# A fused clustered-attention kernel: cluster ties through a triangular matmul, and the first lots and the first head in another order

## The chip, the cores and the metric

The program runs on one core of a Trainium2 chip. TensorE (PE), VectorE (DVE), ScalarE (ACT), GpSimd (POOL) and the sync engine (SP, which here only issues DMAs) each work through a queue of their own, in order, and wait for one another through semaphores. The metric is the device time of one execution in microseconds (us). The kernel before took 671.68 us, the median of three runs (670.71 to 671.84).

## The reference

Three stages in a row: attention of 2 batches x 8 heads x 768 tokens x 64, in which a query sees only the keys of its own cluster, and two MLPs over all 1536 tokens. Only the first stage is touched:

```python
q_assign = np.argmax(np.einsum('bhsd,hcd->bhsc', q_n, c_n), axis=-1)
k_assign = np.argmax(np.einsum('bhsd,hcd->bhsc', k_n, c_n), axis=-1)
mask = q_assign[:, :, :, None] == k_assign[:, :, None, :]
scores = scale * np.matmul(q, k.transpose(0, 1, 3, 2))
scores = np.where(mask, scores, -1000000000.0)
...   # softmax over the keys, then attn @ v, then the two MLPs
```

There are 16 clusters (C) for each head. `argmax` takes the first of equal values, so ties must be resolved the same way.

## The kernel before

Setup. The similarities of all tokens to the 16 centroids of their head are worked out in eight lots. Lot e belongs to batch e // 4, to q (x = 0) or k (x = 1), and to one half of the 768 tokens (c), for all 8 heads at once: 8 heads x 16 clusters fill the 128 partitions. A lot goes round the engines: SP loads it (`load_pairs`, 768 KB), PE multiplies it with the centroids (`sims_of`), ACT copies the result to SBUF (`copy_sims`), PE transposes it so that tokens lie on partitions (`tokens_of`), DVE takes each head's maximum over the 16 and marks who reaches it (`compare`), POOL multiplies the marks with a falling rank (`rank_lot`), DVE takes the maximum rank and marks the winner (`choose`). PE then turns two lots back at a time, clusters on partitions (`hots_of`), and ACT copies them into `hot_t` and scales them (`store_clusters`): 0 or 1 for q, 0 or -2^100 for k. These 16 rows per head are appended to q and k as extra contraction rows, so that the scores of pairs in different clusters become hugely negative.

A head. Each head's k and q (384 KB) are loaded (`load_kq`), scaled on POOL (`scale_q`), rounded to fp32r on ACT (`kq_high`), the remainder is taken on POOL (`kq_low`), and SP moves the parts to their partitions with small SBUF-to-SBUF DMAs (`place_head`): two out of `k_high`, one out of `k_low`, one within `k_high`, and last two with the cluster rows. When the last three have landed (`qk_ready`), PE may start on that head. For head 0 the cluster rows come straight from `hot_t`; for every other head they go through `mask_rows` in DRAM.

Attention. Two heads make a pair of 12 steps, one for each 128 query tokens; eight pairs follow one another, the first written out, the others in a loop. In step n PE makes the scores (`scores_of`, two banks in turn), DVE the row maximum (`row_max`), ACT the exponential (`exps`), POOL the normalisation, and five or six steps later PE transposes the result (`turn`), ACT and DVE split it (`turned_high`, `turned_low`), and PE multiplies it with v. In pair 0 the steps 0 to 5 have no such later work yet. The last two lots' `choose`, the last two `hots_of` and their `store_clusters` stand in steps 0 to 5 of pair 0, at the steps that `CHOOSE_STEPS`, `HOT_STEPS` and `STORE_STEPS` name. Before the first `turn` in step 6, PE waits until `hot_t` is complete, because the transposed probabilities use the same PSUM banks.

The order on each engine is the order in which the code is written; no scheduler moves anything.

Of the kernel before, what the change touches and what calls it, by code (L numbers as in the profile page):

```python
# [16 lines left out]
def clustered_attention_two_mlps(nc, q_t, k_t, v_r, cent, w_gelu, w_ln, gains, out):  # L17
# [32 lines left out]
    with ExitStack() as ctx:  # L50
# [32 lines left out]
        first_rank_i = sb("first_rank_i", [P, C], I32, cluster)  # L83
        first_rank = sb("first_rank", [P, C], F32, cluster)
# [6 lines left out]
        CHOICE_LAG = 1  # L91
        RANKS = CHOICE_LAG + 2
        sims_max = [sb(f"sims_max{r}", [P, CH * H], F32, cluster) for r in range(RANKS)]
        rank_max = [sb(f"rank_max{r}", [P, CH * H], F32, cluster) for r in range(RANKS)]
        rank = [sb(f"rank{r}", [P, HALF], F32, cluster) for r in range(RANKS)]
        hot = [sb(f"hot{x}", [P, S], F32, cluster) for x in range(2)]
        hot_t = [sb(f"hot_t{x}", [P, S], F32, cluster) for x in range(2)]
# [51 lines left out]
        sims_t_ps = [banks[:, 2 * x:2 * x + 2, 0:HALF] for x in range(2)]  # L149
        sims = [banks[:, 4 + c, 0:HALF] for c in range(2)]  # L150
        hot_ps = banks[:, 6:8, 0:HALF]
# [30 lines left out]
        ranked = sem("ranked")  # L182
        rank_max_done = sem("rank_max_done")
        hot_done = sem("hot_done")
        hot_ps_done = sem("hot_ps_done")
# [107 lines left out]
        KQ_STEP, STORE_STEPS, HOT_STEPS, CHOOSE_STEPS = 0, (2, 4), (3, 5), (0, 1)  # L293
# [42 lines left out]
        def _(sp):  # L336
            sp.dma_start(c_raw[:], cent).then_inc(cent_loaded, 16)
            sp.dma_start(gains_sb[:], gains).then_inc(gains_loaded, 16)

# [30 lines left out]
            def place_head(it, j):  # L370
# [16 lines left out]
                move(q_high[j][low, :], k_high[j][high, :], high_moved[j])  # L387
                if isinstance(it, int) and it == 0 and j == 0:

                    load_pairs(LOTS - 1)  # L390
                sp.wait_ge(kq_low_done, (h + 1) * 2)
                move(q_parts[j][high, :], k_low[j][high, :], low_moved[j])
# [23 lines left out]
            for j in range(2):  # L416
                load_v(0, j)
# [46 lines left out]
        def _(pe):  # L464
# [31 lines left out]
            def hots_of(g):  # L496
                pe.wait_ge(hot_done, (g + 1) * 2)
                if g >= 1:

                    pe.wait_ge(hot_t_done, g)  # L500
# [1046 lines left out]
```

## Time and profile before

| what | value |
|---|---|
| median of three runs | 671.68 us |
| profiled execution | 670.98 us, of it 669.1 us span |
| PE busy | 631.0 us (94%) |
| DVE / ACT / POOL busy | 485.1 / 325.1 / 494.1 us |
| first scores of pair 0 | 30.63 us after the start |
| first `turn` (step 6) of pair 0 | 42.57 us |
| first scores of pair 1 | 56.97 us |
| a pair in the middle of the loop | 27.3 us |

The profile gives, for one execution, when each instruction began, how long it took and what ended the idle time of its engine before it. All times are counted from the start of the span. The profiled execution's own time is 1.9 us above its span, for start and end. Everything from pair 1 on is untouched by the change, so the first 57 us decide.

### The profile page before, as it was taken

How to read it: one execution, taken by the hardware profiler on the slowest of the kernel's cores; microseconds unless marked ns; L12 is line 12 of the kernel's file. 1: busy time of each engine (PE TensorE's matmuls, PEld its weight loads, DVE VectorE, ACT ScalarE, POOL GpSimd, SP SyncE). 2: the span in 40 equal slices, each digit the busy share in tenths (PEclk: the TensorE clock that was granted, in tenths of full speed). 3: DMA queues.
4: the chain of work that ended last, by engine and by line, in shares of the span. 5: the costliest groups of instructions: out<-in, count | busy, mean ns of one | idle time of the engine just before them, and what ended most of it. 6: DMA issues, size and time to landing. Idle time of an engine off the chain costs nothing.

```text
span 669.1 us, 11407 instructions
## 1 busy us (share of the span) xinstructions
PE 631.0 (94%) x3245; PEld 528.5 (79%) x3245; DVE 485.1 (72%) x819; ACT 325.1 (49%) x647; POOL 494.1 (74%) x680
## 2 busy tenths in 40 slices
PE   4579999999999999999999999999999999999998
PEld 1369989898989888788877777788888877888876
DVE  3779999999999985666647667755555587778650
ACT  1279999999999984222222222132222243443341
POOL 2677788798888886888879888988887777567000
PEclk9889999999999999999999999999999999999999
DMA  8866544544545421232222222222220000000001
GB/s 283 266 176 145 158 120 112 143 123 126 143 112 137 134 88 64 72 110 88 106 96 82 84 88 91 94 95 96 94 94 31 1 0 17 32 17 17 31 33 47
DMA packets 26936, 64.31 MB, mean 96 GB/s; under 512 B 3872, under 2 KB 10016, under 8 KB 26912
## 3 DMA queue, kind: packets, MB, share of 16 engines
q1 hardware_dynamic: 24896, 60.09, 30.2%
q10 hardware_dynamic: 2016, 3.93, 1.6%
q8 instruction: 11, 0.18, 0.1%
q14 instruction: 13, 0.11, 0.1%
HBM read 46.60 MB, written 4.72 MB: 77 GB/s over the span
## 4 chain that ended last, share of the span: by engine, by line
PE 66%; ACT 11%; DVE 8%; issue 7%; DMA 4%; POOL 2%; DVEq 1%; SPq 1%; ACTq 0%; POOLq 0%
PE banks L560 6%; PE banks L575 6%; PE banks L577 6%; PE banks L590 6%; PE banks L576 6%; PE banks L592 6%; PE banks L591 6%; ACT probs L799 4%; PE banks L545 4%; PE banks L715 3%; PE banks L714 3%; PE banks L713 3%; ACT probs_th L810 2%; PE banks L682 2%; PE banks L684 2%
## 5 line engine op out<-in xcount | busy, mean ns | idle before, releaser
L1028 DVE TENSOR_TENSOR probs_tl<-banks,probs_th 128x384 fp32r<-128x384 f32 x192 | 100.4, 546 | 11.7 <-ACT probs_th L810 9.2
L1008 DVE TENSOR_REDUCE neg_max<-banks 128x1 f32<-128x768 f32 x96 | 91.0, 948 | 10.2 <-PE banks L532 8.4
L810 ACT CAST probs_th<-banks 128x384 fp32r<-128x384 f32 x192 | 83.0, 485 | 21.4 <-PE banks L545 20.0
L1337 POOL TENSOR_TENSOR wait_scrap<-half_power 128x1 f32<-128x1 f32 x176 | 47.2, 268 | 61.4 <-DVE row_inv L1022 29.6
L799 ACT ACTIVATE probs<-banks,neg_max 128x768 f32<-128x768 f32 x96 | 88.1, 918 | 7.6 <-DVE neg_max L1008 7.5
L1002 DVE TENSOR_TENSOR gl<-gate,gh 128x512 fp32r<-128x512 f32 x48 | 43.8, 912 | 65.1 <-ACT gh L784 65.1
L1413 POOL TENSOR_SCALAR probs<-probs,row_inv 128x768 f32<-128x768 f32 x96 | 87.7, 914 | 0.0
L545 PE MATMUL banks<-ident,probs 128*128 128x128 f32 x576 | 79.0, 272 | 0.9 <-ACT hot_t L753 0.9
L560 PE MATMUL banks<-probs_th,v_parts 128*128 128x384 f32 x192 | 70.3, 366 | 9.9 <-DVE x_sums L1035 9.9
L784 ACT CAST gh<-gate 128x512 fp32r<-128x512 f32 x48 | 29.8, 621 | 99.8 <-PE banks L592 58.7
L575 PE MATMUL banks<-xh,uph 128*128 (+1 forms) x192 | 76.7, 400 | 1.0 <-POOL upl L1386 0.8
L1396 POOL TENSOR_TENSOR downl<-gelu_raw,downh 128x512 fp32r<-128x512 f32 x48 | 73.8, 1537 | 4.0
L590 PE MATMUL banks<-gh,downh 128*128 128x512 f32 x192 | 75.9, 395 | 0.2
L577 PE MATMUL banks<-xh,upl 128*128 (+1 forms) x192 | 75.4, 392 | 0.0
L592 PE MATMUL banks<-gh,downl 128*128 128x512 f32 x192 | 75.3, 392 | 0.0
L576 PE MATMUL banks<-xl,uph 128*128 (+1 forms) x192 | 75.1, 391 | 0.0
L591 PE MATMUL banks<-gl,downh 128*128 128x512 f32 x192 | 74.8, 390 | 0.0
L545 PEld LDWEIGHTS banks<-ident,probs 128*128 128x128 f32 x576 | 68.5, 140 | 5.2 <-ACT hot_t L753 1.2
L1386 POOL TENSOR_TENSOR upl<-gelu_raw,uph 128x512 fp32r<-128x512 f32 x48 | 67.7, 1410 | 4.0
L780 ACT ACTIVATE gate<-banks 128x512 f32<-128x512 f32 x48 | 28.8, 599 | 84.8 <-PE banks L577 65.4
L560 PE MATMUL banks<-probs_tl,v_parts 128*128 128x384 f32 x192 | 65.1, 339 | 0.0
L528 PE MATMUL banks<-k_high,q_parts 128*128 128x384 f32 x192 | 56.4, 376 | 5.4 <-DMA k_low<-mask_rows 2.1
(147 smaller groups left out, 1410.7 us busy)
## 6 DMA issues: line engine op xcount, KB each, us to landing
gelu_raw<-w_gelu SPq DMA_DIRECT2D x48, 512.0 KB, 3.3
ln_raw<-w_ln SPq DMA_DIRECT2D x8, 512.0 KB, 4.7
pair_t<-q_t SPq DMA_DIRECT2D x4, 768.0 KB, 7.4
pair_t<-k_t SPq DMA_DIRECT2D x4, 768.0 KB, 8.3
kq_raw<-k_t SPq DMA_DIRECT2D x16, 192.0 KB, 3.7
kq_raw<-q_t SPq DMA_DIRECT2D x16, 192.0 KB, 3.9
q_parts<-k_high SPq DMA_DIRECT2D x16, 192.0 KB, 2.6
q_high<-k_high SPq DMA_DIRECT2D x16, 192.0 KB, 3.0
```

What stands on the lines that cost most here:

```text
L545: last = nc.tensor.transpose(pt_bank(n, c)[:, t * P:(t + 1) * P], probs[:, n % NP, k * P:(k + 1) * P], ident[:])
L560: last = nc.tensor.matmul(head_out, v_parts[j][:, i // 2].rearrange("p two d -> p (two d)"), part[half % 2][:, i // 2, :], start=i == 0, s ...
L575: nc.tensor.matmul(hidden[u], uph[u][:, cols], xh[:, k, tok], start=k == 0, stop=False)
L576: nc.tensor.matmul(hidden[u], uph[u][:, cols], xl[:, k, tok], start=False, stop=False)
L577: last = nc.tensor.matmul(hidden[u], upl[u][:, cols], xh[:, k, tok], start=False, stop=k == KT - 1)
L590: nc.tensor.matmul(acc[d], downh[u][:, cols], gh[u][:], start=first, stop=False)
L591: nc.tensor.matmul(acc[d], downh[u][:, cols], gl[u][:], start=False, stop=False)
L592: last = nc.tensor.matmul(acc[d], downl[u][:, cols], gh[u][:], start=False, stop=end)
L799: nc.scalar.activation(probs[:, n % NP, :].rearrange("p (c t) -> p c t", c=2), scores[n % 2], ACT.Exp, bias=neg_max[:, n % NP:n % NP + 1], ...
L810: nc.scalar.copy(probs_th[half % 2][:, c * CH:(c + 1) * CH, i * P:(i + 1) * P], pt_bank(n, c).rearrange("p (t s) -> p t s", t=CH)).then_in ...
L1008: nc.vector.tensor_reduce(out=neg_max[:, col], in_=scores[n % 2], op=ALU.max, axis=mybir.AxisListType.XY, negate=True).then_inc(max_done, 1)
L1028: nc.vector.tensor_tensor(probs_tl[half % 2][at], pt_bank(n, c).rearrange("p (t s) -> p t s", t=CH), probs_th[half % 2][at].bitcast(F32), ...
```

## The change

Three things, all in the setup and in pair 0.

Ties. The ranks go. The marks of `compare` (now `ties`) are transposed by PE lot by lot (`ties_of`), copied by ACT with a cast to fp32r (`copy_ties`), and multiplied on PE with a constant 128x128 matrix (`first_of`), which for each cluster takes its own mark minus the marks of the earlier clusters of its head (and the negative of it for k). DVE then makes `hot_t` out of that product with one comparison and one scale (`choose`). `hot_t` has a buffer of its own for each batch.

Order of the setup. k and q of heads 0 and 1 are loaded between the lots; `kq_high` of both and the splits on POOL stand amid the first batch's lots; both heads of pair 0 take their cluster rows straight from `hot_t`; the loads of lots 5, 6 and 7 stand inside and behind head 0's moves; the gains are loaded later.

Pair 0. Before it stand the lots 0 to 3 complete, and lot 4 up to its `compare`. The rest of lot 4 and the lots 5, 6, 7 stand in its steps 0 to 5, by the tables of steps. `sims_of` of these lots writes to the banks of `sims`, since the scores have the others.

```diff
-        KQ_STEP, STORE_STEPS, HOT_STEPS, CHOOSE_STEPS = 0, (2, 4), (3, 5), (0, 1)
+        SIMS_STEP = {5: 0, 6: 2, 7: 3}
+        TOKENS_STEP = {5: 0, 6: 3, 7: 4}
+        TIES_STEP = {4: 0, 5: 1, 6: 4, 7: 5}
...
@@ sync: place_head
-                    if isinstance(it, int) and it == 0 and j == 0:
-                        sp.wait_ge(hot_t_done, x + 1)
-                        src = hot_t[x][0:C, :]
+                    if isinstance(it, int) and it == 0:
+                        sp.wait_ge(hot_t_done, 2 * (x + 1))
+                        src = hot_t[0][x][j * C:(j + 1) * C, :]
...
                 move(q_parts[j][high, :], k_low[j][high, :], low_moved[j])
+                if isinstance(it, int) and it == 0 and j == 0:
+                    load_pairs(5)
...
-            for e in range(4):
+            for e in range(2):
                 load_pairs(e)
             load_kq(0, 0)
-            for e in range(4, LOTS - 1):
+            for e in range(2, 4):
                 load_pairs(e)
             load_kq(0, 1)
+            sp.dma_start(gains_sb[:], gains).then_inc(gains_loaded, 16)
+            load_pairs(4)
             place_head(0, 0)
...
+            for e in range(6, LOTS):
+                load_pairs(e)
             for j in range(2):
                 load_v(0, j)
+            place_head(0, 1)
             load_kq(1, 0)
             for x in range(2):
-                sp.wait_ge(mask_stored[x], 16)
-            place_head(0, 1)
+                sp.dma_start(mask_rows[x, 0], hot_t[0][x][:]).then_inc(mask_stored[x], 16)
+            for x in range(2):
+                sp.wait_ge(hot_t_done, 4 + 2 * (x + 1))
+                sp.dma_start(mask_rows[x, 1], hot_t[1][x][:]).then_inc(mask_stored[x], 16)
@@ tensor
+            def ties_of(e):
+                pe.wait_ge(compared, e + 1)
+                if e >= 1:
+                    pe.wait_ge(ties_t_copied, e)
+                for i in range(CH):
+                    last = nc.tensor.transpose(ties_ps[:, i * P:(i + 1) * P], ties[e % 2][:, i * P:(i + 1) * P],
+                                               ident[:])
+                last.then_inc(ties_done, 1)
+            def first_of(e):
+                x = e // 2 % 2
+                pe.wait_ge(ties_t_copied, e + 1)
...
+                    pe.wait_ge(hot_t_done, e)
+                nc.tensor.matmul(first_ps, first_w[x][:], ties_t[e % 2][:], start=True, stop=True
+                                 ).then_inc(first_done, 1)
...
-                        pe.wait_ge(hot_t_done, LOTS // 2)
+                        pe.wait_ge(hot_t_done, LOTS)
@@ scalar
+            def copy_ties(e):
+                act.wait_ge(ties_done, e + 1)
+                if e >= 2:
+                    act.wait_ge(first_done, e - 1)
+                nc.scalar.copy(ties_t[e % 2][:], ties_ps).then_inc(ties_t_copied, 1)
@@ vector: choose
+                dve.wait_ge(first_done, e + 1)
+                nc.vector.tensor_scalar(hot_t[b][x][:, c * HALF:(c + 1) * HALF], first_ps, float(x), -FAR if x else 1.0,
+                                        ALU.is_ge, ALU.mult).then_inc(hot_t_done, 1)
@@ gpsimd
-            def rank_lot(e):
...
+            def first_weights():   # two affine_select and two subtractions, 128x128 each
...
+            first_weights()
+            scale_q(0, 0)
+            for c in range(2):
+                kq_low(0, 0, c)
+            scale_q(0, 1)
```

TensorE, the head of pair 0, before (the digit behind a name is its buffer; `banks` is PSUM, L528 and L532 are the scores, L502 is `hots_of`):

```order
L528 MATMUL banks<-k_high0,q_parts0 128x384 [waits qk_ready0]
L528 MATMUL banks<-k_high0,q_parts0 128x384
L532 MATMUL banks<-k_low0,q_high0 128x384 x2
L528 MATMUL banks<-k_high0,q_parts0 128x384 x2
L532 MATMUL banks<-k_low0,q_high0 128x384 x2
L528 MATMUL banks<-k_high0,q_parts0 128x384 [waits exp_done0]
L528 MATMUL banks<-k_high0,q_parts0 128x384
L532 MATMUL banks<-k_low0,q_high0 128x384 x2
L502 MATMUL banks<-ident,hot0 128x128 [waits hot_t_done,hot_done]
L502 MATMUL banks<-ident,hot0 128x128 x5
```

The same place in the changed kernel (L561 and L565 are the scores, L516 `ties_of`, L529 `first_of`, L493 `sims_of`, L505 `tokens_of`):

```order
L561 MATMUL banks<-k_high0,q_parts0 128x384 [waits qk_ready0]
L561 MATMUL banks<-k_high0,q_parts0 128x384
L565 MATMUL banks<-k_low0,q_high0 128x384 x2
L516 MATMUL banks<-ident,ties0 128x128 [waits ties_t_copied,compared]
L516 MATMUL banks<-ident,ties0 128x128 x2
L529 MATMUL banks<-ties_t0,first_w0 128x384 [waits hot_t_done,ties_t_copied]
L493 MATMUL banks<-pair_t0,c_diag 32x384 [waits compared,pair_loaded0_1]
L493 MATMUL banks<-pair_t0,c_diag 32x384 x3
L505 MATMUL banks<-ident,sims_t0 128x128 [waits compared,sims_t_copied]
L505 MATMUL banks<-ident,sims_t0 128x128 x2
L561 MATMUL banks<-k_high0,q_parts0 128x384 x2
L565 MATMUL banks<-k_low0,q_high0 128x384 x2
```

Between the scores of step 0 and those of step 1 there now stand four pieces of the lots 4 and 5, two of which wait for a copy on ACT.

ScalarE, where pair 0 begins, before (L799 is `exps`, L766 `kq_high`, L753 `store_clusters`):

```order
L799 ACTIVATE probs,row_sum<-banks,neg_max 128x768 [waits max_done]
L766 CAST k_high1<-kq_raw1 128x768 [waits q_scaled]
L799 ACTIVATE probs,row_sum<-banks,neg_max 128x768 [waits max_done] x2
L753 ACTIVATE hot_t0<-banks 128x768 [waits qk_ready0,mask_stored0,hot_ps_done]
L757 DMA mask_rows<-hot_t0 128x768 [waits hot_t_done]
```

The same place in the changed kernel (L837 is `exps`, L790 `copy_ties`, L783 `copy_sims`):

```order
L837 ACTIVATE probs,row_sum<-banks,neg_max 128x768 [waits max_done]
L790 CAST ties_t0<-banks 128x384 [waits first_done,ties_done]
L783 COPY sims_t0<-banks 128x384 [waits sims_done,sims_t_done]
L837 ACTIVATE probs,row_sum<-banks,neg_max 128x768 [waits max_done]
L790 CAST ties_t1<-banks 128x384 [waits first_done,ties_done]
```

The copies that TensorE waits for stand behind the exponential of their step.

The sync engine, the placing of head 0, before:

```order
L375 DMA q_parts0<-k_high0 64x768 [waits kq_high_done]
L375 DMA q_high0<-k_high0 64x768
L347 DMA pair_t1<-k_t 128x4x384 [waits sims_t_done]
L375 DMA q_parts0<-k_low0 64x768 [waits kq_low_done]
L375 DMA k_high0<-k_high0 64x768 [waits high_moved0]
L383 DMA q_high0<-hot_t0 16x768 [waits hot_t_done,low_moved0]
L383 DMA k_low0<-hot_t1 16x768 [waits hot_t_done]
```

And in the changed kernel:

```order
L382 DMA q_parts0<-k_high0 64x768 [waits kq_high_done]
L382 DMA q_high0<-k_high0 64x768
L382 DMA q_parts0<-k_low0 64x768 [waits kq_low_done]
L354 DMA pair_t0<-q_t 128x4x384 [waits sims_t_done]
L382 DMA k_high0<-k_high0 64x768 [waits high_moved0]
L390 DMA q_high0<-hot_t0_0 16x768 [waits hot_t_done,low_moved0]
L390 DMA k_low0<-hot_t0_1 16x768 [waits hot_t_done]
```

The lot loaded among the moves is now lot 5 and stands behind the move out of `k_low0`; before it was lot 7 and stood ahead of it.

## Rows read from the trace of the kernel before

**Rows 1.** The page: span, busy time, one group (busy us, mean ns, idle)

```profile
span 669.1 us, 11407 instructions
PE 631.0 (94%) x3245; PEld 528.5 (79%) x3245; DVE 485.1 (72%) x819; ACT 325.1 (49%) x647; POOL 494.1 (74%) x680
...
L560 PE MATMUL banks<-probs_tl,v_parts 128*128 128x384 f32 x192 | 65.1, 339 | 0.0
```

**Rows 2.** Chain of waits around the first scores of pair 0: start, duration, what

```profile
22.50 4.97 DMA q_parts<-k_low
...
28.10 2.48 DMA k_low<-hot_t
30.63 1.01 PE banks L528 x2
31.64 0.65 PE banks L532 x2
...
42.55 4.63 DMA mask_rows<-hot_t
```

**Rows 3.** Timeline of the first lots: start, duration, instruction, idle before

```profile
6.33 1.51 PE L479 MATMUL banks<-pair_t,c_diag 128*32 128x384 f32 x8 [1.71 <-DMA pair_t<-q_t]
...
7.89 0.48 ACT L743 COPY sims_t<-banks 128x384 f32<-128x384 f32 x1 [5.87 <-PE banks L479]
...
8.36 1.51 PE L479 MATMUL banks<-pair_t,c_diag 128*32 128x384 f32 x8 [0.52 <-DMA pair_t<-q_t]
...
9.80 0.90 PE L491 MATMUL banks<-ident,sims_t 128*128 128x128 f32 x3
...
11.33 0.56 DVE L970 TENSOR_TENSOR rank<-banks,sims_max 128x384 f32<-128x384 f32 x1
...
12.00 0.55 PE L491 MATMUL banks<-ident,sims_t 128*128 128x128 f32 x3
...
12.87 0.85 PE L479 MATMUL banks<-pair_t,c_diag 128*32 128x384 f32 x8 [0.32 <-DMA pair_t<-k_t]
...
16.49 0.85 PE L479 MATMUL banks<-pair_t,c_diag 128*32 128x384 f32 x8 [1.62 <-DMA pair_t<-q_t]
...
26.55 0.85 PE L479 MATMUL banks<-pair_t,c_diag 128*32 128x384 f32 x8 [1.75 <-DMA pair_t<-k_t]
```

**Rows 4.** Timeline of pair 0

```profile
32.39 0.96 DVE L1008 TENSOR_REDUCE neg_max<-banks 128x1 f32<-128x768 f32 x1 [2.65 <-PE banks L532]
...
33.38 0.90 ACT L799 ACTIVATE probs<-banks,neg_max 128x768 f32<-128x768 f32 x1 [5.43 <-DVE neg_max L1008]
...
40.70 0.62 PE L528 MATMUL banks<-k_high,q_parts 128*128 128x384 f32 x2 [0.25 <-ACT probs L799]
...
41.16 0.52 PE L532 MATMUL banks<-k_low,q_high 80*128 80x384 f32 x2
...
42.57 0.88 PE L545 MATMUL banks<-ident,probs 128*128 128x128 f32 x6 [0.89 <-ACT hot_t L753]
...
44.99 0.62 PE L528 MATMUL banks<-k_high,q_parts 128*128 128x384 f32 x2 [1.55 <-DMA k_low<-mask_rows]
...
56.97 0.61 PE L528 MATMUL banks<-k_high,q_parts 128*128 128x384 f32 x2 [0.55 <-DMA k_low<-mask_rows]
```

**Rows 5.** Windows: stretch, busy time by engine, granted clock, DMA share, GB/s

```profile
9.30:12.70 3.40, 3.25 (x18) 1.01 (x14) 1.23 (x3) 0.96 (x2) 0.65 (x1) 1.00 1.08 352
...
15.40:18.80 3.40, 1.73 (x14) 0.80 (x14) 3.30 (x7) 0.04 (x1) 2.36 (x3) 1.00 1.06 372
...
25.60:29.00 3.40, 1.40 (x11) 0.47 (x11) 2.50 (x5) 0.48 (x1) 1.46 (x2) 0.99 0.58 139
...
29.00:29.50 0.50, 0.00 (x0) 0.00 (x0) 0.47 (x2) 0.00 (x0) 0.00 (x0) 0.50 0.07 19
...
35.80:39.20 3.40, 3.40 (x13) 2.91 (x12) 2.42 (x5) 2.19 (x5) 3.05 (x6) 0.50 0.74 158
...
39.20:39.60 0.40, 0.40 (x4) 0.40 (x3) 0.40 (x1) 0.00 (x0) 0.40 (x2) 1.00 0.69 154
```

More of the change, by code:

```diff
@@ L90, in clustered_attention_two_mlps @@
         LOTS = 4 * B
[L91 to L97, printed above, removed]
+        LATE_LOT = LOTS - 3
+        sims_max = [sb(f"sims_max{r}", [P, CH * H], F32, cluster) for r in range(2)]
+        ties = [sb(f"ties{r}", [P, HALF], F32, cluster) for r in range(2)]
+        ties_t = [sb(f"ties_t{r}", [P, HALF], F32R, cluster) for r in range(2)]
+        earlier = sb("earlier", [P, P], F32, cluster)
+        first_w = [sb(f"first_w{x}", [P, P], F32R, cluster) for x in range(2)]
+        hot_t = [[sb(f"hot_t{b}_{x}", [P, S], F32, cluster) for x in range(2)] for b in range(B)]
         cluster.close()
@@ L635, in attention_turn @@
                             head_half(*lagged(it, n, lag, STEPS), c)
+                    for e in range(4, LOTS):
+                        if first and TIES_STEP[e] == n:
+                            ties_of(e)
+                        if first and FIRST_STEP[e] == n:
+                            first_of(e)
+                        if first and SIMS_STEP.get(e) == n:
+                            sims_of(e)
+                        if first and TOKENS_STEP.get(e) == n:
+                            tokens_of(e)
                     if drain and n in UP_STEPS:
@@ L766, in kq_high @@
                 nc.scalar.copy(k_high[j][:], kq_raw[j][:]).then_inc(kq_high_done, 1)
-            for e in range(LOTS):
-                copy_sims(e)
-                if e == 3:
-                    kq_high(0, 0)
-                if e in (4, 5):
-                    store_clusters(e - 4)
+            copy_sims(0)
+            copy_sims(1)
+            copy_ties(0)
+            kq_high(0, 0)
+            copy_sims(2)
+            copy_ties(1)
+            copy_sims(3)
+            copy_ties(2)
+            copy_ties(3)
+            kq_high(0, 1)
+            copy_sims(4)
             def gelu(at, u):
@@ L980, in choose @@
-                dve.wait_ge(rank_max_done, e + 1)
-                if g >= 2:
-                    dve.wait_ge(hot_ps_done, g - 1)
-                nc.vector.tensor_tensor(heads(hot[x][:, c * HALF:(c + 1) * HALF]), ranks,
-                                        most[:].unsqueeze(2).to_broadcast([P, G, C]),
-                                        ALU.is_equal if x else ALU.not_equal).then_inc(hot_done, 1)
-            for b in range(B):
-                for e in range(4 + CHOICE_LAG):
-                    if e < 4:
-                        compare(b * 4 + e)
-                    if e >= CHOICE_LAG and b * 4 + e - CHOICE_LAG < LOTS - len(CHOOSE_STEPS):
-                        choose(b * 4 + e - CHOICE_LAG)
+                b, x, c = e // 4, e // 2 % 2, e % 2
@@ L1043, in attention_turn @@
                         row_max(it, n)
-                    if isinstance(it, int) and it == 0 and n in CHOOSE_STEPS:
-                        choose(LOTS - len(CHOOSE_STEPS) + CHOOSE_STEPS.index(n))
+                    for e in range(4, LOTS):
+                        if isinstance(it, int) and it == 0 and CHOOSE_STEP[e] == n:
+                            choose(e)
+                        if isinstance(it, int) and it == 0 and COMPARE_STEP.get(e) == n:
+                            compare(e)
                     if pair:
```

157 lines of the change are left out of this document (74 added, 83 removed).

## The prediction

> **What bounds the kernel now.** I read the page first, for where time can be won at all; then the chain of waits through the first 57 us, for what sets the start of attention; then the timeline of that stretch, for the price of each piece; last the windows with TensorE's clock. The page shows PE busy for 94% of the span [rows 1]. The reader is to see that the change doesn't touch this long part: from pair 1 on nothing moves, so the result is how much earlier or later pair 1 begins than at 56.97 us [rows 4].
>
> The chain shows what sets the first scores of head 0, at 30.63: not the cluster rows' arithmetic but a small move, `q_parts<-k_low`, issued at 22.50 and 4.97 us under way, and behind it the last two small moves, 2.48 us [rows 2]. Why 4.97 us: the 768 KB of lot 7 were issued ahead of it on the same queue, and PE got them only at 26.55 [rows 3]. The timeline of pair 0 shows two more waits: step 6's `turn` at 42.57 waited 0.89 us for `hot_t`, and step 6's scores at 44.99 waited 1.55 us for head 1's cluster rows from `mask_rows`. Pair 1's scores waited 0.55 us for theirs [rows 4].
>
> **Term 1, the first scores come earlier.** The prices [rows 3], at full clock: `sims_of` 0.85, `tokens_of` or `ties_of` (three transposes) 0.55, an ACT copy 0.48, a handover 0.05 (PE ends at 7.84, ACT starts at 7.89), each pass of `compare` 0.56. At half clock `sims_of` is 1.51 and three transposes 0.90. `choose` is one pass over PSUM now: 0.56 as its neighbour, where two passes and a POOL multiplication stood. `first_of` isn't in this trace; its nearest row is one fp32r matmul of 128x384, 0.34 alone [rows 1]; between 0.2 (its successor starts under it) and 0.7 (twice that, at half clock). I work with both 0.34 and 0.2 and take the middle.
>
> The gains' load leaves the head of the queue and gives 0.46 us: lot 0 is on PE at 5.9. In order on PE, with a copy on ACT between nearly all pieces: lot 0's and 1's `sims_of` and `tokens_of` at half clock with two copies end at 11.9; `ties_of(0)`, copy, `first_of(0)` at 13.3. A lot after that is 0.85 + 0.58 + 0.55 + 0.55 + 0.58 + 0.34 = 3.45, or 3.3 with 0.2. Two of them end at 19.9 to 20.2; `ties_of(3)`, copy, `first_of(3)`, `choose(3)` add 1.9 to 2.1. The cluster rows of k stand ready between 21.8 and 22.3, and their DMA is 2.48 behind that [rows 2]: 24.3 to 24.8. The handovers inside a lot (two of the 0.05 lie under the copies' own ends) take off up to 0.5; I take 24.3, bounds 23.7 to 24.9.
>
> The data don't hold this up. Two lots arrive in 12.87 - 8.36 = 4.5, a lot in 2.25 (PE waited for both, lots 1 and 3 [rows 3]); a head's k and q in 16.49 - 12.87 - 2.25 = 1.4, a small move in half of that, 0.7. Lot 1 at 7.9, head 0 at 9.3, lots 2 and 3 at 13.8, head 1 at 15.2, lot 4 at 17.4, three moves at 19.5, lot 5 at 21.8, the move within `k_high` at 22.5: before 24.3. The splits of head 0 on POOL and ACT have from 9.3 to 17.4. That cover is thin: if a lot took 3.1 us to arrive, this queue would be last. The matrix for `first_of` (four POOL instructions of 128x128) is made while POOL waits for head 0.
>
> So the first scores gain 30.63 - 24.3 = 6.3 us.
>
> **Term 2, steps 0 to 5 of pair 0 get longer.** Before, from 30.63 to the first `turn` at 42.57 it was 11.9 us [rows 4]. Now lots 5 to 7 stand in them. What counts isn't the sum of their work, but that engines in order wait for one another. In us from the first scores, at full clock: scores 0.98 (40.70 to 41.68), row maximum to 1.98, exponential to 2.91 [rows 4]. `copy_ties(4)` stands behind that exponential on ACT, to 3.4; PE waits for it with `first_of(4)` and everything queued behind, `sims_of(5)`, a copy again, `tokens_of(5)`, and only then the scores of step 1, at 5.6. Before they followed step 0's at once. Then: `compare(5)` is ahead of step 1's maximum on DVE (7.8), its exponential 8.7, `copy_ties(5)` 9.2, `first_of(5)` and `sims_of(6)` 10.3, scores of step 3 at 11.3, `tokens_of(6)` and `sims_of(7)` 12.7, scores of step 4 at 13.7, their maximum and exponential 15.5, `copy_ties(6)` 16.0, `first_of(6)` and `tokens_of(7)` 16.9, `compare(7)` 18.0, `ties_of(7)`, copy, `first_of(7)`, `choose(7)` 20.0. The `turn` of step 6 waits for exactly that. 20.0 against 11.94 costs 8.0 us; with Term 1 the first `turn` comes at 44.3, 1.7 later than before. Bounds of this length: the work alone, without the waits, is 15.1 (below); with the most that half clock adds (1.4 in step 0, 1.6 behind it, both below) it is 23.0.
>
> **Term 3, what is given back behind it.** Head 1's rows no longer go through DRAM: their moves are issued around 32, and the 1.55 us before step 6's scores go. Not all counts, since ACT's own queue lay beside: between 0 and 1.55, I take 0.7. At pair 1's start the 0.55 goes between not at all and in full. `hot_t` is complete 1.7 later; its way through DRAM took 4.63 with other loads ahead [rows 2], now it stands ahead of them. I take 0.4.
>
> What else moves on the queues costs nothing by this count: behind head 0's rows SP issues lots 6 and 7 (4.5 us, landed near 28, first needed by `sims_of(6)` at about 33.8), v, head 1's six moves (to about 34, needed at 45) and head 2's k and q (near 36; POOL scales them behind step 2's normalisation, about 43). Each has 5 us of cover; where it ends, POOL and the transposes behind it would be late by what is missing.
>
> **Term 4, the clock.** The granted clock fell to half at 29 us, after 3.4 us in which PE was busy for 1.40, and came back at 39.2 after 3.4 us without a gap; with 1.73 of 3.4 busy it had stayed [rows 5]. In the new order PE has nothing between `tokens_of(4)`, about 22.7, and 24.3, then 1.5 us of work up to `ties_of(4)`, and waits to 27.6. That is 1.5 busy in about 4.9 us, as thin as before the fall. So I expect half clock from step 0's wait on: then `tokens_of(5)`, scores 1 and 2 and `ties_of(5)` cost 0.35 + 0.68 + 0.68 + 0.35 more (scores take 1.66 [rows 2] for 0.98), part of it under ACT and DVE, and leave no gap on PE, which brings the clock back. 0.9, between 0 and 1.6.
>
> The Trainium skill ("TensorE: Matmul & The Clock Gate", HAM oscillation) has it that only a single idle gap of PE longer than a bound drops the clock. The trace disagrees: no single wait before 29 us was longer than 1.75 [rows 3], and it fell. By the page no wait in pair 0 is long enough, and the term would be 0 (the second rival).
>
> **The sum.** -6.3 + 8.0 - 0.7 - 0.4 + 0.9 = +1.5. Against the profiled execution of 670.98 that is 672.5. It lay 0.70 below the median of the runs shown, so I forecast 671.68 + 1.5 = 673.2.
>
> **The rivals.**
>
> Lots at half clock (slower): three transposes took 0.90 at 9.80 and 0.55 at 12.00 [rows 3], so the engine came to full speed between the two, whatever the column of the granted clock says, after a stretch in which it was busy for 3.25 of 3.4 us [rows 5]. The new order puts a copy between each two pieces, and I count 2.9 busy in the same stretch. If it doesn't rise there, lots 2 and 3 run at half: two `sims_of` 1.32, two `tokens_of` 0.7, four `ties_of` 1.4, four `first_of` 1.0, together 4.4, and step 0 another 1.4 (scores 0.68, `sims_of` 0.66). +1.5 + 4.4 + 1.4 = +7.3: 679.0. For it speaks the count, against it that at half clock the pieces themselves fill the engine. It decides as soon as `tokens_of(2)` takes 0.90.
>
> The clock stays full in pair 0: Term 4 is nothing, +0.6: 672.3. It has the skill's rule for it and the fall at 29 us against it.
>
> The waits of pair 0 overlap: each engine works through its sum. PE up to `tokens_of(7)` is 5 x 0.98 + 3 x 0.55 + 3 x 0.34 + 3 x 0.85 + 3 x 0.55 = 11.8, the last lot's tail 3.3: 15.1 instead of 20.0, hence 1.5 - 4.9 = -3.4: 668.3. For it: my counting adds each handover and no reordering of weight loads. Against it: the copies stand behind exponentials that themselves wait for scores. It decides if scores 1 begin within 3.5 us of scores 0, which at 5.6 I don't see.
>
> The queue stays last: if the small moves wait for lot 5 as they did for lot 7, Term 1 loses 2.25 and the sum is +3.7: 675.4.
>
> **How the numbers follow.** The forecast 0.40 (its own range 671.8 to 674.6), half-clock lots 0.10, full clock 0.15, overlap 0.30 (with what lies half way), the queue 0.05. A measurement of this kernel tells about 0.2%, 1.3 us, from no change. The forecast stands just at that bound, so its 0.40 go 0.21 slower, 0.16 same, 0.03 faster; with the two slow rivals 0.15, full clock 0.02 slower, 0.09 same, 0.04 faster, and overlap 0.26 faster, 0.04 same: slower 0.38, same 0.29, faster 0.33. The range is 668.0 to 676.5; it leaves out the half-clock lots and what would beat a full overlap.
>
> **What would show it.** The profile after should have the first scores at 24.3, scores 1 some 5.6 later (6 or more at half clock), the first `turn` at 44 to 45, no wait for `mask_rows` before step 6, pair 1's scores at 58.5, and from there on the same 27.3 us a pair. Term 1 is wrong if the first scores come after 26, Term 2 if the first `turn` comes less than 17 us behind them. Were the clock full between 26 and 36, Term 4 is. The forecast as a whole is wrong if pair 1 starts before 57.0.

## The result: 0.98% slower, and the profile after

The changed kernel takes 677.49 us, the median of six runs (675.99 to 680.75), where the kernel before took 671.76 (670.71 to 672.59) on the same chip: ratio 1.0098, 95% interval 1.0074 to 1.0122. The forecast was 673.2 with a range up to 676.5, so it was wrong, and on the slow side. The profiled execution took 680.75, the slowest of the six: the traces have to tell of 9.8 us, the medians of 5.7. (The quotient of the two medians is 1.0085; the ratio on record isn't that quotient.)

The page of the changed kernel (span, busy time; the last row answers to the group of [rows 1]: busy us, mean ns, idle):

```profile
span 679.0 us, 11429 instructions
PE 644.1 (95%) x3253; PEld 535.7 (79%) x3253; DVE 480.4 (71%) x810; ACT 325.4 (48%) x651; POOL 485.9 (72%) x676
...
L593 PE MATMUL banks<-probs_tl,v_parts 128*128 128x384 f32 x192 | 65.1, 339 | 0.0
```

PE is 13 us busier though only eight matmul instructions were added; the timelines below show the same pieces at a lower speed. The product with v, all of it in the loop, costs what it did. So the place is ahead of the loop, and the timeline of the first lots answers to [rows 3] (start, duration, instruction, idle time before it and what ended it):

```profile
8.02 0.90 PE L505 MATMUL banks<-ident,sims_t 128*128 128x128 f32 x3 [0.59 <-ACT sims_t L783]
...
13.07 0.69 PE L529 MATMUL banks<-ties_t,first_w 128*128 128x384 f32 x1 [0.57 <-ACT ties_t L790]
13.69 1.51 PE L493 MATMUL banks<-pair_t,c_diag 128*32 128x384 f32 x8
15.79 0.90 PE L505 MATMUL banks<-ident,sims_t 128*128 128x128 f32 x3 [0.60 <-ACT sims_t L783]
...
18.52 1.51 PE L493 MATMUL banks<-pair_t,c_diag 128*32 128x384 f32 x8
...
27.36 0.90 PE L505 MATMUL banks<-ident,sims_t 128*128 128x128 f32 x3 [0.60 <-ACT sims_t L783]
28.06 1.01 PE L561 MATMUL banks<-k_high,q_parts 128*128 128x384 f32 x2
```

At 15.79 `tokens_of(2)` still takes 0.90: the sign that the prediction named for its rival "Lots at half clock". It takes 0.90 at 27.36 too. Before, three such transposes took 0.55 from 12.00 on [rows 3]. In what follows "full speed" and "half speed" are 2.4 and 1.2 GHz, told by such durations. `first_of` takes 0.69 at half speed, which is about the 0.7 that the prediction set as its upper bound. The first scores come at 28.06 with no wait ahead of them: no transfer ended last, PE's own pieces did.

The timeline of pair 0, against [rows 4]:

```profile
32.22 0.69 PE L529 MATMUL banks<-ties_t,first_w 128*128 128x384 f32 x1 [1.81 <-ACT ties_t L790]
...
35.50 0.99 PE L561 MATMUL banks<-k_high,q_parts 128*128 128x384 f32 x2
...
44.88 0.62 PE L561 MATMUL banks<-k_high,q_parts 128*128 128x384 f32 x2
...
48.30 0.69 PE L529 MATMUL banks<-ties_t,first_w 128*128 128x384 f32 x1 [2.11 <-ACT ties_t L790]
...
53.68 1.54 PE L578 MATMUL banks<-ident,probs 128*128 128x128 f32 x6 [0.65 <-DVE hot_t L1014]
54.87 0.99 PE L561 MATMUL banks<-k_high,q_parts 128*128 128x384 f32 x2
...
67.10 0.61 PE L561 MATMUL banks<-k_high,q_parts 128*128 128x384 f32 x2
```

The second scores stand 7.44 us behind the first (before: 32.08, 1.45 behind). Twice PE waited about 2 us for a copy of ties that stood behind an exponential on ACT. The scores take 0.62 (full speed) at 44.88 only, and 0.99 again from 49.28 on.

The windows that answer to [rows 5] (stretch, PE busy, granted clock, DMA share, GB/s):

```profile
9.30:12.70 3.40, 2.60 (x14) 1.00 1.06 367
...
15.40:18.80 3.40, 2.44 (x11) 1.00 1.08 312
25.60:29.00 3.40, 2.80 (x14) 1.00 0.32 55
35.80:39.20 3.40, 3.40 (x12) 1.00 0.43 93
40.20:43.60 3.40, 3.40 (x16) 1.00 0.85 273
44.00:47.40 3.40, 2.19 (x15) 1.00 0.35 139
48.00:51.40 3.40, 3.10 (x11) 0.50 0.00 0
```

The column of the granted clock says 1.00 down to 47.40, and up to 43.9 it is wrong: the durations are those of 1.2 GHz. In the stretch in which PE was 3.25 us busy before it is 2.60 busy now, and the clock didn't come up. It did at 43.9, when PE had had a single gap of 0.30 us since 34.95, and it was down again by 48.3.

In the table, "first" is the first scores, "pair 0" the time from there to the first `turn`, "pair 1" the start of its scores, "rest" the profiled execution's own time less pair 1. Each kernel was timed in one of four sets, beside the kernel before on the same chip; the medians of the latter were 671.76 (for the changed kernel), 672.67 (1 to 4), 672.63 (5 to 8) and 672.67 (9 and 10). So compare ratios first, and medians of two kernels by how far each is from its own of these.

| kernel | median | ratio to before (95%) | first | pair 0 | pair 1 | rest |
|---|---|---|---|---|---|---|
| before | 671.76 | 1 | 30.63 | 11.94 | 56.97 | 614.0 |
| changed | 677.49 | 1.0098 (1.0074-1.0122) | 28.06 | 25.62 | 67.10 | 613.7 |
| 1 filled start | 676.49 | 1.0062 (1.0042-1.0081) | 24.88 | 24.49 | 62.08 | 613.0 |
| 2 filled throughout | 673.74 | 1.0023 (1.0008-1.0038) | 26.14 | 21.19 | 60.06 | 613.8 |
| 3 before, filled | 674.59 | 1.0027 (1.0012-1.0041) | 34.45 | 10.94 | 60.55 | 614.0 |
| 4 lots out | 670.08 | 0.9974 (0.9959-0.9988) | 27.84 | 8.90 | 56.95 | 612.9 |
| 5 reordered, filled | 669.46 | 0.9955 (0.9937-0.9973) | 29.82 | 14.14 | 57.12 | 612.9 |
| 6 and queue | 669.86 | 0.9961 (0.9944-0.9977) | 28.53 | 13.81 | 56.09 | 612.4 |
| 7 before, queue | 672.39 | 1.0001 (0.9984-1.0018) | 32.81 | 11.64 | 60.57 | 614.0 |
| 8 reordered, unfilled | 671.51 | 0.9993 (0.9979-1.0007) | 30.00 | 15.34 | 59.16 | 613.8 |
| 9 copies ahead | 674.45 | 1.0025 (1.0011-1.0038) | 28.38 | 19.89 | 61.38 | 612.4 |
| 10 fewer fills | 667.66 | 0.9926 (0.9901-0.9952) | 26.99 | 14.18 | 54.77 | 612.9 |

The last column settles where to look: it stays within 1.6 us over twelve kernels, while pair 1 moves over 12.3.

### The profile page after: what moved, and what is told of

It reads as the page before. It is cut to its first block, busy times and chain, and to the rows that moved or that the text cites. A ratio compares the mean times of both kernels' runs of the same rounds, so it can differ in the third digit from the quotient of the medians.

```text
span 679.0 us, 11429 instructions
## 1 busy us (share of the span) xinstructions
PE 644.1 (95%) x3253; PEld 535.7 (79%) x3253; DVE 480.4 (71%) x810; ACT 325.4 (48%) x651; POOL 485.9 (72%) x676
## 4 chain that ended last, share of the span: by engine, by line
PE 70%; ACT 11%; DVE 8%; issue 7%; POOL 1%; DVEq 1%; DMA 1%; ACTq 0%; POOLq 0%; SPq 0%
PE banks L593 7%; PE banks L608 6%; PE banks L610 6%; PE banks L609 6%; PE banks L623 6%; PE banks L625 6%; PE banks L624 6%; PE banks L578 5%; ACT probs L837 4%; ACT probs_th L848 3%; PE banks L755 2%; PE banks L753 2%; PE banks L754 2%; PE banks L722 2%; PE banks L724 2%
## 5 line engine op out<-in xcount | busy, mean ns | idle before, releaser
L837 ACT ACTIVATE probs<-banks,neg_max 128x768 f32<-128x768 f32 x96 | 88.3, 920 | 10.8 <-DVE neg_max L1040 10.8
L561 PE MATMUL banks<-k_high,q_parts 128*128 128x384 f32 x192 | 57.3, 381 | 0.0
```

Source lines behind the costliest of these rows:

```text
L837: nc.scalar.activation(probs[:, n % NP, :].rearrange("p (c t) -> p c t", c=2), scores[n % 2], ACT.Exp, bias=neg_max[:, n % NP:n % NP + 1], ...
```

## The experiments

The theory after the result had three parts: TensorE's clock in setup and pair 0, the order of the pieces in pair 0, and the DMA queue as what stands behind both. A "fill" is a matmul of the identity with itself (128x128), whose result nobody reads, put where PE would wait; in a profile it shows as two records (x18 are nine fills).

### 1. Fills ahead of the first lot only

```diff
+            fill(9, 3)     # 9 matmuls, ahead of the centroids' transpose
...
+            fill(6, 3)     # 6 more, before the wait for c_diag
```

> The changed kernel with 15 idle matmuls (identity by identity, into a free bank) on TensorE before lot 0, and nothing else. Theory A (the clock): the change lost because TensorE, with a copy on ScalarE between each two pieces, never reached full clock in the setup; brought up before lot 0 it stays up as it did in the kernel before, tokens_of(2) takes 0.55 instead of 0.90, the first scores come near 24.3 instead of 28.1, and the time is 672 to 674. Theory B (the waits): what cost is the order of pair 0, whatever the clock; the first scores come earlier but the time falls by less than 4 us minus what pair 0 takes back, to 673.5 or more, and pair 0 still takes over 24 us to its first turn. Theory C (more work on TensorE): within 1 us of 677.5.

The first scores came at 24.88 instead of 28.06. The lots ran at full speed from the first on, until about 20. Its timeline of PE (`sims_of(2)`, `tokens_of(2)`, `sims_of(3)`, `first_of(3)`, `sims_of(4)`):

```profile
13.19 0.85 PE L501 MATMUL banks<-pair_t,c_diag 128*32 128x384 f32 x8
14.64 0.55 PE L513 MATMUL banks<-ident,sims_t 128*128 128x128 f32 x3 [0.60 <-ACT sims_t L791]
...
16.46 0.85 PE L501 MATMUL banks<-pair_t,c_diag 128*32 128x384 f32 x8
...
20.82 0.69 PE L537 MATMUL banks<-ties_t,first_w 128*128 128x384 f32 x1 [0.57 <-ACT ties_t L798]
21.43 1.51 PE L501 MATMUL banks<-pair_t,c_diag 128*32 128x384 f32 x8
```

Its windows:

```profile
9.30:12.70 3.40, 2.21 (x17) 1.00 1.06 362
15.40:18.80 3.40, 2.22 (x17) 1.00 1.08 314
20.90:24.30 3.40, 2.80 (x12) 0.50 0.83 221
```

In the stretch of 9.30 to 12.70 PE was less busy than in the changed kernel (2.21 for 2.60) and kept 2.4 GHz, where the other stayed at 1.2: the state that it comes in with matters. It isn't all, for the clock fell by 20.8 with the pieces as before and no wait above 0.60 us, and in experiment 4 it rose among the very pieces that kept the changed kernel at half speed. Fifteen matmuls of no use are worth 3.2 us here, though they hold `sims_of(0)` back from 5.92 to 8.00. Pair 0 still took 24.49, at half speed until about 41. So theory B was the better one: theory A had the time at 672 to 674.

### 2. Fills in all of PE's waits in the lots and in pair 0

```diff
+                fill(3 if e < 6 else 0, {3: 2, 5: 4}.get(e, 3))      # in tokens_of
+                fill({4: 12, 5: 4, 6: 12}.get(e, 3), ...)            # in first_of
+                        fill(8, 3)                                   # before the first scores
+                        fill(3, 5)                                   # before the first turn
```

> The changed kernel with idle matmuls before lot 0 and ahead of every wait of TensorE in the lots and in steps 0 to 6 of pair 0 (3 to 12 each, by the length of the wait). Theory A: full clock throughout, first scores at 24.3, first turn 20 us later at 44.3, pair 1 near 57.3, time 672.3. Theory B: the same 20 us to the first turn, and so no gain on the kernel before in spite of the full clock; if the order alone were harmless the first turn would come at 40 and the time near 668. Theory C: time above 675.

PE ran at full speed from the first lot to pair 1, which began 7.0 us earlier; the median fell by 3.8 (4.7, each set against its own kernel before). This measures the order without the clock: pair 0 takes 21.19 us (forecast 20.0), the second scores stand 5.9 behind the first (32.03; forecast 5.6). Even so the kernel isn't faster than the one before, as theory B had it. And now a transfer ends last at the first scores, as the chain of waits shows (start, duration, what):

```profile
13.12 1.97 POOL k_low L1396 x2
...
15.10 7.27 DMA q_parts<-k_low
...
23.00 3.09 DMA k_low<-hot_t
...
26.14 0.62 PE banks L573 x2
```

The small move out of `k_low` took 7.27 us, more than the 4.97 before [rows 2], with lot 4 and head 1 issued shortly ahead of it; that these are the reason is argued, not tested.

### 3. Fills in the kernel before

```diff
+                if e == 7:
+                    fill(12, 2)    # and 3 behind it
...
+                        fill(16, 2)    # before the first scores
```

> The kernel before with idle matmuls in TensorE's waits between 24 and 31 us (12 before the last lot, 3 before its tokens, 16 before the first scores), so that the clock does not fall at 29. Theory A: the fall cost the kernel before something as well, in steps 0 to 3; but step 6 waits for the cluster rows of head 1 through DRAM in any case, so the gain is 0 to 1 us: 670.8 to 671.8. If it is faster by over 2 us, the waits for DRAM weren't what held pair 0.

A miss. Its timeline of PE: `tokens_of` and `sims_of` of the lots ahead of the first fill, then the 12 fills, the 16 fills and the first scores:

```profile
20.50 0.59 PE L500 MATMUL banks<-ident,sims_t 128*128 128x128 f32 x3 [1.31 <-ACT sims_t L754]
21.03 1.51 PE L486 MATMUL banks<-pair_t,c_diag 128*32 128x384 f32 x8
...
26.30 2.84 PE L469 MATMUL banks<-ident 128*128 128x128 f32 x24
...
30.96 3.74 PE L469 MATMUL banks<-ident 128*128 128x128 f32 x32
34.45 0.60 PE L539 MATMUL banks<-k_high,q_parts 128*128 128x384 f32 x2
```

The first scores came 3.8 us late. The fills ran at full speed (0.12 us a record, as in experiment 2), but there were too many. `k_low<-hot_t` was issued at 28.48; with the 2.48 of [rows 2] it landed near 31.0, an estimate, and PE was through with lot 7 at 31.1, so the 16 fills had no wait left to fill. That PE was so late has two parts: the 12 fills outlasted their wait (2.84 for 1.75), and PE was 1.7 us late already when the first fill began, since the clock had fallen at about 21 and came back at 24.4. In the trace of the kernel before the same code kept full speed there: one kernel's clock isn't the same in every execution. One more thing can be read: with the clock up, the old pair 0 takes 10.94 instead of 11.94, so the half speed in it had cost about 1.0.

### 4. The lots out of pair 0

```diff
-        SIMS_STEP = {5: 0, 6: 2, 7: 3}
...
+        NONE = {4: -1, 5: -1, 6: -1, 7: -1}
+        SIMS_STEP = TOKENS_STEP = TIES_STEP = ... = NONE
```

> The changed kernel with the rest of lot 4 and the lots 5 to 7 left out (the second batch uses the clusters of the first): measures what they cost in pair 0. The setup is as in the changed kernel, at half clock, first scores at 28.1. All theories: first turn 12 us later, near 40, time near 668. Theory B then has the whole rest (13 us in the profiled execution at half clock, 8 at full) as the price of the lots in pair 0; if the first turn still comes 16 us or more behind the first scores, something else in pair 0 is slow.

The second batch takes the first batch's clusters here, so the kernel leaves out the rest of lot 4 and the lots 5 to 7. Pair 0 fell to 8.90 us (expected 12), the first `turn` came at 36.74 (near 40); but pair 1 began at 56.95, as before the change, and the time was 2 us above the 668 expected. A transfer stood in the way twice, as the timeline shows at the scores of step 6 and of pair 1:

```profile
40.63 1.01 PE L555 MATMUL banks<-k_high,q_parts 128*128 128x384 f32 x2 [2.41 <-DMA k_low<-hot_t]
...
56.95 0.61 PE L555 MATMUL banks<-k_high,q_parts 128*128 128x384 f32 x2 [0.89 <-DMA k_low<-mask_rows]
```

In its chain `q_parts<-k_low` of head 1, issued at 29.92, was 7.88 us under way behind lots 6, 7 and v; head 2's k and q were issued at 47.34, behind the wait for the mask rows. So the queue is a second floor: however short pair 0 was, pair 1 began no earlier than in the kernel before. That it would be about 57 for any short pair 0 in this order is argued from this one trace. By the medians, each against its own kernel before (+5.7 and -2.6), the lots in pair 0 cost 8.3 us, and the rest of the change saves 2.6.

Nothing ahead of pair 0 was changed here, so its first lots are those of the changed kernel once more. They began at half speed too, but came up (`ties_of(2)`, `first_of(2)`, `ties_of(3)`):

```profile
21.90 0.85 PE L510 MATMUL banks<-ident,ties 128*128 128x128 f32 x3
23.31 0.44 PE L523 MATMUL banks<-ties_t,first_w 128*128 128x384 f32 x1 [0.57 <-ACT ties_t L784]
23.60 0.49 PE L510 MATMUL banks<-ident,ties 128*128 128x128 f32 x3
```

In the changed kernel `first_of(2)` took 0.69, as it did in experiments 8 and 9, which have the same first lots. So in one of four traces the clock came up amid those gaps. How often it does in the executions behind a median isn't known.

### 5. Another order in pair 0, with fills in the setup

T, K, F, S are `ties_of` (on ACT `copy_ties`), `tokens_of`, `first_of`, `sims_of` (on ACT `copy_sims`); C and H `compare` and `choose`; the digit is the lot.

```diff
+        PE_STEPS = {0: "T4 K5", 1: "F4 S6 T5", 3: "K6 F5 S7", 4: "T6", 5: "K7 F6 T7 F7"}
+        ACT_AHEAD = {0: "T4", 4: "T6"}                    # ahead of the exponential
+        ACT_BEHIND = {1: "S6 T5", 3: "S7", 4: "T7"}
+        DVE_STEPS = {0: "C5", 1: "H4", 3: "C6 H5", 5: "C7 H6 H7"}
...
+            sims_of(5)                                    # ahead of pair 0
```

> The changed kernel with fills in the setup and with the lots' pieces in the first pair put in another order: similarities of lot 5 before the pair, each piece on TensorE at a step where the copy or the comparison that it waits for has had a step's time, the copies of ties to SBUF ahead of the exponentials in steps 0 and 4. Theory (in pair 0 the order costs, since a piece waits behind exponentials of 1.4 us each): first `turn` 14 to 16 us after the first scores instead of 21.2 (all fills) or 25.6 (none), so at about 41; and by the theory on the queue it gives back little behind that, since head 2's move waits for the mask rows of both batches as in the run that left the lots out: pair 1's scores at 57 to 58, time about 670 (ratio to before 0.997). Rival (only the clock costs, the order costs nothing): first `turn` still 21 us after the first scores and 673.7 as with all fills. Rival (pieces cost their own durations wherever they stand): 20 us, 673.

Pair 0 took 14.14 us, where 14 to 16 were expected, and the kernel is 0.45% faster than the one before. The first scores came only at 29.82, since `sims_of(5)` waited 2.62 us for its load and eight fills then stood ahead of them, which took 3.45 us at half speed. Pair 1 began at 57.12 as expected.

### 6. The same, and head 2's moves freed from the second batch's mask rows

```diff
@@ sync
-                sp.dma_start(mask_rows[x, 1], ...)     # now on ScalarE's queue, step 6
+            for x in range(2):
+                sp.wait_ge(mask_stored[x], 16)         # the first batch's rows only
+            place_turn(1)
```

> The run before this one, and in the DMA queue of SyncE: the mask rows of the second batch are stored from ScalarE's queue in step 6, and head 2's moves are issued as soon as the first batch's rows lie, without a wait for the second's. Theory (the queue's wait for the mask rows is the second floor): pair 1's scores at 52 to 54, four to five us ahead of the kernel before, and a time of 666 to 668 (ratio 0.992). Rival (the first pair's own work on TensorE sets pair 1's scores): within 1 us of the run before this one, 669 to 670. Rival (ScalarE's stores in step 6 stop exponentials behind them until VectorE has transposed the hot rows): slower than the run before this one by 1 to 2 us.

The theory on the queue (666 to 668) missed, and the rival with 669 to 670 held: no gain in the medians (669.86 for 669.46). Pair 1 began 1.03 earlier, but so did the first scores (1.29; the eight fills ahead of them took 2.05 us here): from the first `turn` to pair 1 it took 13.75 instead of 13.16. Head 2's k and q were issued at 42.39 instead of 46.87, the rows in `k_low` at 54.02 instead of 54.57. Behind the load the moves wait for the splits that ACT and POOL make: the first was issued at 46.04 and the one out of `k_low` at 49.22, and this one was 4.39 us under way.

### 7. The kernel before, with only the queue changed

```diff
                 sp.wait_ge(kq_low_done, (h + 1) * 2)
                 move(q_parts[j][high, :], k_low[j][high, :], low_moved[j])
+                    load_pairs(LOTS - 1)      # was ahead of that wait
...
+            place_turn(1)                     # ahead of the wait for batch 2's rows
```

> The kernel before with only the DMA queue changed: lot 7's load issued behind the moves that the first scores wait for, and head 2's moves issued before the wait for the second batch's mask rows. Theory (in the kernel before as well the queue ends last at the first scores): first scores at 29.0 to 29.8 instead of 30.63, pair 1's scores without their wait of 0.55, time 670.2 to 671 (ratio 0.998). Rival (lot 7's load comes last instead, and moves lot 7's pieces back by as much as the scores gain): ratio 1.000. The kernel does all its work.

The rival held: 1.0001. Lot 7's load was now last. It was issued at 23.56, its similarities ran at 30.15, and the scores behind them on PE came at 32.81, later than before. This profiled execution (674.56) was its slowest; by the median nothing was lost.

### 8. The other order alone, without fills

The edit is that of experiment 5 without its fills.

> The changed kernel with the pieces of pair 0 in the other order and no fills at all: tells order from clock. Theory (both cost, in sum): first scores at 28 as in the changed kernel, first `turn` 17 to 20 us after them instead of 25.6, time 672 to 674 (ratio 1.002). Rival (the clock alone costs): first `turn` 25 us after the first scores and 677. Rival (the order alone costs): 15 us, and 670.

Pair 0 took 15.34 us, less than the 17 to 20 expected and next to the 15 of the rival that the order alone costs; the kernel is as fast as the one before (0.9993). The clock came back at 33.6, 10 us earlier than in the changed kernel; this order left PE no gap from 28.56 on (the window's columns as above; L568 is the second half of the scores, 0.84 at half speed):

```profile
30.00:33.40 3.40, 3.40 (x17) 1.00 1.05 378
```

The timeline around it:

```profile
33.37 0.65 PE L568 MATMUL banks<-k_low,q_high 80*128 80x384 f32 x2
...
35.64 0.52 PE L568 MATMUL banks<-k_low,q_high 80*128 80x384 f32 x2
```

So order and clock aren't two separate costs: without fills the clock costs pair 0 only 15.34 - 14.14 = 1.2 us in this order, where it cost 25.62 - 21.19 = 4.4 in the changed one.

### 9. Three copies moved ahead of an exponential

```diff
+                    for e in (4, 5, 6):
+                        if isinstance(it, int) and it == 0 and COPY_TIES_STEP[e] == n:
+                            copy_ties(e)
                     if not drain:
                         exps(it, n)
```

> The changed kernel with one thing moved: ScalarE's copies of the ties of lots 4, 5 and 6 stand ahead of the exponentials of steps 0, 1 and 4 instead of behind them. Tells how much of pair 0's 25.6 us is the wait behind an exponential. Theory (the in-order copy is one of the two large waits): TensorE's waits for these copies fall from 1.81, 0.30 and 2.11 us to about 0.6, 0.3 and 0.6, first `turn` 2.5 to 3 us earlier after the first scores (22.5 to 23), time 674.5 to 675 (ratio 1.006). Rival (what holds pair 0 is where the pieces stand on TensorE, between its scores; the exponential then ends later by what the copy takes): within 1 us of the changed kernel, 677.

Nothing else differs from the changed kernel. Pair 0 fell from 25.62 to 19.89 us, further than the 22.5 to 23 expected; the median fell by 3.0 us to 674.45 (3.95, each against its own kernel before), where 674.5 to 675 was expected. Its timeline (L529 `first_of`, L493 `sims_of`, L561 the scores):

```profile
31.29 0.69 PE L529 MATMUL banks<-ties_t,first_w 128*128 128x384 f32 x1 [0.57 <-ACT ties_t L790]
...
38.59 1.18 PE L493 MATMUL banks<-pair_t,c_diag 128*32 128x384 f32 x8
39.71 0.62 PE L561 MATMUL banks<-k_high,q_parts 128*128 128x384 f32 x2
...
43.92 0.44 PE L529 MATMUL banks<-ties_t,first_w 128*128 128x384 f32 x1 [0.57 <-ACT ties_t L790]
```

The two waits of 1.81 and 2.11 are 0.57 each: 2.8 us. The other 2.9 are left to the clock, which rose at 38.6 instead of 43.9 and stayed up; that the moved copies brought it up earlier is argued.

### 10. Experiment 6 without the fills ahead of the first scores

```diff
-                    if isinstance(it, int) and it == 0 and j == 0:
-                        fill(8, 3)
```

> The reordered kernel with the changed queue, without the eight fills that stood ahead of the first scores: there they no longer filled a wait (lot 5's similarities had taken its place) and pushed the scores back. Theory (pair 0 starts and ends earlier by what the fills took): first scores at 26.8 to 27.4 instead of 28.5, first `turn` at 41, pair 1's scores at 55 to 56, time 668 to 669.5 (ratio 0.995). Rival (pair 1's scores are held by head 2's moves in the queue, issued at 54): pair 1's scores at 56, no change against the run with them. Rival (the clock falls without them): first `turn` as before or later.

The timeline of PE: lot 5's similarities, the first scores and the first `turn`.

```profile
25.25 0.85 PE L504 MATMUL banks<-pair_t,c_diag 128*32 128x384 f32 x8 [1.19 <-DMA pair_t<-q_t]
26.99 0.62 PE L575 MATMUL banks<-k_high,q_parts 128*128 128x384 f32 x2 [0.89 <-DMA k_low<-hot_t]
...
41.17 1.54 PE L592 MATMUL banks<-ident,probs 128*128 128x128 f32 x6 [0.65 <-DVE hot_t L1022]
```

The fastest of all: 667.66 us, ratio 0.9926 (0.9901 to 0.9952), 1.5% under the changed kernel, and a little better than the 668 to 669.5 expected. The scores wait for transfers again (0.89), and pair 1 begins at 54.77, below the 57 of experiment 4. Whether the queue's part is needed for that wasn't tried: the order without it was run with all fills (experiment 5) or with none (8).

## Why the prediction was wrong

**What bounds it** held. Nearly everything is decided before pair 1; behind it all kernels agree within 1.6 us. In the trace pair 1 began 10.1 us later than before, where the sum had 1.5. Of the 8.6 missing, Term 1 has 3.7, Term 4 has 3.5 and Term 2 has 1.2; the first two are TensorE's clock. The medians moved by 5.7 only, and no trace tells how the miss divides there.

**Term 1**, first scores at 24.3 (bounds 23.7 to 24.9): the step that failed. Its count gave a lot 3.45 us on PE at full clock; in the changed kernel a lot took 18.52 - 13.69 = 4.83, and the first scores came at 28.06. In experiment 1, with the clock up until 20, a lot took 16.46 - 13.19 = 3.27, and the scores came at 24.88. The arithmetic was right, the clock was assumed: I took the 0.55 of [rows 3] for all lots, though these came behind 3.25 us of work in 3.4 [rows 5], and my own count of the new order had 2.9 there. It was 2.60. I set against the rival that at half speed the pieces would fill the engine. They don't, since the copy between them, 0.48 and two handovers, doesn't scale with PE's clock: each is a gap of 0.57 to 0.60. Not all of it was to be had by counting: by the trace of experiment 4 the same lots can also come up, at about 23.

**"The data don't hold this up"** was true in the changed kernel, where PE was later than the queue. It is false as soon as PE is fast: 1.49 us of wait for `k_low<-hot_t` in experiment 2, 0.89 in experiment 10. I had put 0.7 us on a small move, from the rate at which loads arrive; the one out of `k_low` took 7.27 in experiment 2.

**Term 2**, scores to `turn` 20.0, was right in its mechanism and near in size: 21.19 with the clock up. Its upper bound of 23.0 had 3.0 for half speed in it, and was passed at 25.62, since half speed cost 4.4 (Term 4). Experiment 9 shows the mechanism, experiments 5 and 8 that it was the order and not the work: the same pieces, one of them moved ahead of the pair, fit into 14.1 us with the clock up and 15.3 without fills, about the 15.1 that the prediction gave as the work alone.

**Term 3**, -1.1: from the first `turn` to pair 1's scores it was 14.40 before and 13.42 after, -1.0, though about 4 us of it ran at half speed now, and there was no wait for `mask_rows` before step 6.

**Term 4**, the clock in pair 0, +0.9 (0 to 1.6), measured 25.62 - 21.19 = +4.4. I let the clock return after step 2. It came back at 43.9, fell by 48.3 with the wait of 2.11 us and stayed low to about 58.

**The rivals.** "Lots at half clock" was what happened, at the point named for it (`tokens_of(2)` 0.90) and near its price: 679.0, as a median, for 677.49, and +7.3 for the +9.8 of the trace. That it came so near is in part luck: it had 4.4 for the lots and 2.3 for the clock in pair 0, where the runs have 3.7 and 4.4. I gave it 0.10 and cut the range short of it, against a count of my own that spoke for it. "The clock stays full in pair 0" is refuted. The Trainium skill ("TensorE: Matmul & The Clock Gate", HAM oscillation) gives as its rule that PE should have no idle gap above a certain length, and no wait here is that long; the trace has the clock fall between 45.7 and 48.3, where the longest wait was 2.11, and that of experiment 1 by 20.8, behind waits of 0.60 at most. So a gap of that length isn't needed, and the rule alone can't tell whether the clock holds. "The waits overlap" is refuted for the changed kernel: scores 1 came 7.44 behind. "The queue stays last" came true only where fills had removed the other cause (experiments 2 and 10).

## What to carry to other kernels

Before a full-speed duration is put on a new order, read in the trace behind what work the engine reached that speed, count the new order's gaps, and give the half-speed case a chance that fits the count. A copy that TensorE waits for goes ahead of a long instruction on its engine: three such copies of 0.48 us were worth 3 to 4 us of 677. When two causes stand one behind the other, as PE's pieces and the DMA queue here, removing one alone may show nothing: in experiment 4 pair 0 was 16.7 us shorter and pair 1 began no earlier than in the kernel before. That both together give more isn't shown: experiment 6 had both and gained nothing on experiment 5, and what experiment 10 gained on it (2.2 us) came with eight fills fewer. And one trace is one execution: where the same code runs at half speed in one trace and at full speed in another, take a second trace before a clock is made the cause.

## What the hardware showed that I had not expected

The granted clock of a window can read 1.00 while every duration in it is that of 1.2 GHz (up to 43.9 in the changed kernel); only durations tell. The engine kept 2.4 GHz with 1.73 [rows 5] or 2.21 of 3.4 us busy, and at 1.2 GHz didn't come up with 2.80 (25.60 to 29.00 in the changed kernel). The same code did both: the changed kernel's first lots stayed at 1.2 GHz in three traces and came up in that of experiment 4, and the lots of the kernel before kept 2.4 GHz at 21 us in its own trace and lost it in that of experiment 3. So these rows give no rule. The small move out of `k_low` took 4.39 us from issue to landing in one place (head 2, experiment 6) and 7.88 in another (head 1, experiment 4).

Behind pair 1 the code is the same, but the time isn't. The kernel before and its variants (experiments 3 and 7) take 614.0 there and all the others less. Two of PE's waits go with that: in the loop, 60 to 300 us, it waits 9.9 us in all for `x_sums` of DVE in the first group and 8.7 to 8.9 in the others; and behind 500 us the changed kernel and experiments 2 and 8 (613.7 to 613.8) wait 1.5 us once for `hid` of DVE, where the rest wait 0.6 to 0.7 at that line (612.4 to 613.0). Why either differs is open.

Open too: the changed kernel's own six runs lie 4.8 us apart. A clock that comes up in some executions and not in others, as the traces of the changed kernel and of experiment 4 have it, would do that, but only one of the six was traced.
